# The fourth of each four products of h and its cosine on VectorE instead of GpSimd

## The chip, the cores and the metric

The kernel runs on one core of a Trainium2 chip, in float32 throughout. The metric is the device time of one execution in microseconds (us).

## The reference

Three stages follow one another. Attention keeps, in each row of scores, those that are at least the 32nd largest; its output is the input of a dense layer with a cosine gate; that layer's output goes through a mixture of eight experts, one per token.

```python
# attention: q, k, v are (4, 8, 576, 64)
scores = scale * np.matmul(q, k.transpose(0, 1, 3, 2))
kth = np.partition(scores, -top_k, axis=-1)[..., -top_k:-top_k + 1]   # top_k = 32
scores = np.where(scores >= kth, scores, -1000000000.0)
attn = np.exp(scores - np.max(scores, axis=-1, keepdims=True))
attn = attn / (np.sum(attn, axis=-1, keepdims=True) + 1e-09)
x = np.matmul(attn, v)                 # as (2304, 512)
# dense layer: w_in (512, 2048), w_out (2048, 512)
h = x @ w_in
x = (h * np.cos(h)) @ w_out
# experts: e = argmax(x @ w_gate); out = gate * sigmoid * (relu(x @ w1[e]) @ w2[e])
```

## The kernel before

Every engine has its own program, written out by hand, and they meet at semaphores. The work up to the experts is one loop of 75 steps (`LOOP`, 72 steps and a lag of three). Step `st` makes the scores of one tile of 128 queries for one pair of heads, four steps to a tile; the tiles that straddle two batches (steps 16 to 19 and 52 to 55) are "packed" and cost TensorE more. The stages of one step's data are spread over the following steps:

- in step `st` TensorE makes scores (L927, L933), ScalarE copies them from PSUM (L539), and VectorE finds the 32 largest of each row, for two heads: seven pairs of operations, op 0 to op 6, MAX8 (L728) at the even ones and MATCH_REPLACE8 (L730) at the odd ones;
- in step `st + 1` GpSimd turns the tops into constants (L407), ScalarE marks what lies below them (L525), GpSimd masks (L414, two instructions);
- in step `st + 2` ScalarE takes the exponentials (L533), GpSimd and VectorE make reciprocals of the sums (L419, L735), GpSimd multiplies by them (L424, two instructions);
- in step `st + 3` TensorE transposes the probabilities (L945, L952), ScalarE copies them (L547), TensorE multiplies them by v (L965 to L972), ScalarE copies the result into `x_T`.

Beside this runs the dense layer for the tokens of eight steps before, in blocks of two tiles, `m` = 0 to 7. `block_at(st)` gives the block and its place `i` = `st - (8m + 11)`, 0 to 9, so a block's i = 8 and 9 fall on the next block's i = 0 and 1. At i = 0 to 3 TensorE makes `h_T` (`hidden`, L983, 16 slices of 128 features by 256 tokens), in two parts of a step, with the transposes of the probabilities between them. At i = 2 and 4 VectorE reduces eight slices of h modulo 2 pi, `reduce_h`, in two operations: L743 behind op 1 and L746 behind op 2. ScalarE takes the absolute value (L591) at the end of that step and the sine (L596) in the next, each in two halves. At i = 3 and i = 5 GpSimd multiplies h by its cosine, in four products of two slices each (128 x 512 elements, `gate`, L434): pieces 0 to 3 of half g = 0 at i = 3, of half g = 1 at i = 5. They stand last in GpSimd's step, behind L424. At i = 4 to 7 TensorE multiplies the gated h by w_out (`outputs`, L994): features 0 to 7 of the first tile of tokens at i = 4 and of the second at i = 5, features 8 to 15 at i = 6 and 7, again in two parts of a step. Before every second feature it waits for the piece that holds it.

The last two tiles are done behind the loop in code of their own (L454, L602, L773, L1037, L1047), then come the routing on VectorE and the experts (L1108 to L1136), which the change does not touch.

Of the kernel before, what the change touches and what calls it, by code (L numbers as in the profile page):

```python
# [9 lines left out]
ALU = mybir.AluOpType  # L10
# [48 lines left out]
FULL = NT // BLOCK - 1  # L59
# [4 lines left out]
LAST = (NT - 2, NT - 1)  # L64
# [26 lines left out]
def block_at(s):  # L91

    return [(m, s - (8 * m + 8 + LAG)) for m in range(FULL) if 0 <= s - (8 * m + 8 + LAG) < 10]
# [45 lines left out]
def late_fill(t, quarter):  # L139
    return 4 * (t - LAST[0]) + quarter  # L140


def at_least(eng, sem, value):
    if value > 0:
        eng.wait_ge(sem, value)
# [9 lines left out]
def build(nc, q, k, v, w_in, w_out, w_gate, w_ogate, w1, w2, out):  # L155
# [4 lines left out]
    with ctx:  # L160
        def sb(name, shape, dt=F32, stack=ctx):
            return stack.enter_context(nc.sbuf_tensor(name, shape, dt))

        def sem(name):
            return ctx.enter_context(nc.semaphore(name))
# [59 lines left out]
        HS = sb("h_T", [P, NF, BT], stack=att)  # L225
        R = sb("reduced_h", [P, 2, NF // 2, BT], stack=att)
# [18 lines left out]

        names = ("ld_win ld_wout ld_wg const_ready small_filled small_emptied scores_done scores_copied "
                 "tops_done consts_done below_done masked_done exps_done den_done rden_done probs_ready probsT_done "
                 "probsT_copied dense_filled dense_emptied reduced_done cos_done gated_done late_filled late_emptied "
                 "route_chain sub_ready og_ready route_exp table_ready addr_ready "
                 "table_written rows_ready ids_cleared experts_loaded xgT_filled xgT_copied "  # L250
                 "eh_done relu_done ehT_done ehT_copied slot_done y_scaled tri_done oh_ready "
# [1 line left out]
        s = {n: sem(n) for n in names}  # L253
# [113 lines left out]
        def _(pool):  # L367
# [36 lines left out]
            def consts(u):  # L404
                pool.wait_ge(s["tops_done"], tops_at(u, 1, 6))
                at_least(pool, s["exps_done"], 2 * (u - 2))
                nc.gpsimd.tensor_tensor(TC[:, u % 3, :, :], TOP[:, u % 3, :, 0:TOPK:TOPK - 1],  # L407
                                        factors[:].unsqueeze(1).to_broadcast([P, 2, 2]), ALU.mult).then_inc(s["consts_done"], 1)

            def mask(u, i):  # L410

                pool.wait_ge(s["below_done"], 2 * u + i + 1)
                ex = EX[:, u % 3, i * S:(i + 1) * S]
                nc.gpsimd.tensor_tensor(ex, SS[:, u % 3, i, :], ex, ALU.subtract).then_inc(s["masked_done"], 1)  # L414

            def denominators(u):
                pool.wait_ge(s["exps_done"], 2 * u + 2)
                at_least(pool, s["rden_done"], u - 1)
                nc.gpsimd.tensor_scalar_add(DEN2[:, u % 2, :], DEN[:, u % 3, :], 1e-9).then_inc(s["den_done"], 1)  # L419

            def normalise(u):
                pool.wait_ge(s["rden_done"], u + 1)
                for i in range(2):
                    nc.gpsimd.tensor_scalar(EX[:, u % 3, i * S:(i + 1) * S], EX[:, u % 3, i * S:(i + 1) * S], RD[:, u % 2, i:i + 1], 1.0,  # L424
                                            ALU.mult, ALU.mult).then_inc(s["probs_ready"], 1)

            def gate(st, piece):

                for m, i in block_at(st):
                    if i in (3, 5):  # L430
                        g = (i - 3) // 2
                        f = g * 8 + piece * 2
                        pool.wait_ge(s["cos_done"], m * 8 + 4 * g + 2 + piece // 2 + 1)
                        nc.gpsimd.tensor_tensor(HS[:, f:f + 2, :], HS[:, f:f + 2, :], R[:, g, piece * 2:piece * 2 + 2, :],  # L434
                                                ALU.mult).then_inc(s["gated_done"], 1)

            for st in range(LOOP):
                if 0 <= st - 1 < NS:
                    consts(st - 1)
                if 0 <= st - 2 < NS:  # L440
                    denominators(st - 2)
                if 0 <= st - 1 < NS:
                    mask(st - 1, 0)
                    mask(st - 1, 1)
                if 0 <= st - 2 < NS:
                    normalise(st - 2)
                for piece in range(4):
                    gate(st, piece)

            for t in LAST:  # L450
# [262 lines left out]
        def _(dve):  # L713
            V = nc.vector

            def top_op(u, i, op):

                rnd = op // 2
                top = TOP[:, u % 3, i, rnd * 8:rnd * 8 + 8]
                src = SS[:, u % 3, i, :] if op < 2 else WK[:, i, :]  # L720
                if op == 0:
                    if i == 0:
                        dve.wait_ge(s["scores_copied"], u + 1)
                    at_least(dve, s["consts_done"], u - 2)
                else:
                    dve.wait_ge(s["tops_done"], tops_at(u, i, op - 1))
                if op % 2 == 0:
                    V.max(top, src).then_inc(s["tops_done"], 1)  # L728
                else:
                    V.match_replace(WK[:, i, :], top, src, NEG).then_inc(s["tops_done"], 1)  # L730
# [6 lines left out]
            def reduce_h(m, g, part):  # L737
                hs = HS[:, g * 8:(g + 1) * 8, :].rearrange("p a n -> p (a n)")
                r1 = R[:, g, :, :].rearrange("p a n -> p (a n)")
                if part == 0:  # L740
                    dve.wait_ge(s["dense_emptied"], m * MOE_FILLS + 8 * (g + 1))
                    at_least(dve, s["gated_done"], (2 * (m - 1) + g + 1) * 4)
                    V.tensor_scalar(r1.bitcast(I32), hs, 1.0 / TWO_PI, None, ALU.mult).then_inc(s["reduced_done"], 1)  # L743
                else:
                    dve.wait_ge(s["reduced_done"], m * 4 + 2 * g + 1)
                    V.scalar_tensor_tensor(out=r1, in0=r1.bitcast(I32), scalar=-TWO_PI, in1=hs,  # L746
                                           op0=ALU.mult, op1=ALU.add).then_inc(s["reduced_done"], 1)

            for st in range(LOOP):
                for op in range(7):  # L750
                    for i in range(2):
                        if st < NS:
                            top_op(st, i, op)
                        if op == 2 and i == 1 and 0 <= st - 2 < NS:
                            reciprocals(st - 2)
                    for m, i in block_at(st):
                        if i in (2, 4) and op in (1, 2):
                            reduce_h(m, (i - 2) // 2, op - 1)
# [8 lines left out]
            def late_reduce(t, g):  # L767
                n = FULL * 4 + (t - LAST[0]) * 4 + g * 2
                dve.wait_ge(s["late_emptied"], late_fill(t, 2 * g + 1) + 1)
                dve.wait_ge(s["gated_done"], FULL * 8 if t == LAST[0] else FULL * 8 + 2 * (g + 1))  # L770
                hs = HS[:, g * 8:(g + 1) * 8, t % 2 * P:t % 2 * P + P]
                r = R16[:, g * 8:(g + 1) * 8, :]
                V.tensor_scalar(r.bitcast(I32), hs, 1.0 / TWO_PI, None, ALU.mult).then_inc(s["reduced_done"], 1)  # L773
                dve.wait_ge(s["reduced_done"], n + 1)
                V.scalar_tensor_tensor(out=r, in0=r.bitcast(I32), scalar=-TWO_PI, in1=hs,
                                       op0=ALU.mult, op1=ALU.add).then_inc(s["reduced_done"], 1)
# [112 lines left out]
        def _(pe):  # L889
# [96 lines left out]
            def outputs(m, t, f0):  # L986
                if f0 == 0:
                    pe.wait_ge(s["dense_emptied"], m * MOE_FILLS + NF - 1 + t)
                    if m == 0 and t == 0:
                        pe.wait_ge(s["ld_wout"], 16)  # L990
                for f in range(f0, f0 + 4):
                    if f % 2 == 0:
                        pe.wait_ge(s["gated_done"], 8 * m + f // 2 + 1)
                    last = MM(HO[:, t, :], HS[:, f, t * P:(t + 1) * P], wout[:, f, :], start=f == 0, stop=f == NF - 1)  # L994
                if f0 == NF - 4:
                    last.then_inc(s["dense_filled"], 1)
# [44 lines left out]
            def late_outputs(t, f0):  # L1041
                if f0 == 0:
                    pe.wait_ge(s["dense_emptied"], y_fill(t - 2))
                for f in range(f0, f0 + 8):
                    if f % 4 == 0:
                        pe.wait_ge(s["gated_done"], FULL * 8 + (t - LAST[0]) * 4 + f // 4 + 1)
                    last = MM(HO[:, t % 2, :], HS[:, f, t % 2 * P:t % 2 * P + P], wout[:, f, :], start=f == 0, stop=f == NF - 1)  # L1047
                if f0 == 8:
                    last.then_inc(s["dense_filled"], 1)
# [134 lines left out]
```

## Time and profile before

| | |
|---|---|
| median of three runs | 1360.67 us (1356.54 to 1361.6) |
| the profiled execution | 1360.97 us |
| its span, first to last instruction | 1358.9 us |
| mean granted TensorE clock | 0.955 of full speed |
| TensorE matmuls busy | 1245.0 us, 92% |
| VectorE busy | 851.5 us, 63% |
| ScalarE busy | 641.1 us, 47% |
| GpSimd busy | 554.2 us, 41% |

The profiled execution lies 0.3 us above the median. 2.07 us of it lie outside the span. The loop fills the time from 13 to 869 us; VectorE's share of the whole span is low because it has little to do in the experts, and says nothing of the loop, which has to be read step by step.

### The profile page before, as it was taken

Reading aid. Unit: us, or ns where it says so; the run is one execution under the profiler, and the core shown is the slowest. Engines: PE = TensorE matmul, PEld = TensorE weight load, DVE = VectorE, ACT = ScalarE, POOL = GpSimd, SP = SyncE. Lnnn points to the kernel's source line nnn. Section 1 sums busy time; section 2 is a strip of 40 time slices with the busy share of each in tenths; the row PEclk is TensorE's granted clock in tenths of the full one; section 3 lists DMA queues with packets and bytes.
Section 4 is the critical chain, followed back from the end, with each engine's and each line's share of the span. In section 5 each row is a group of like instructions: output and inputs, shape, how many; then the busy total and the mean of one; then the engine's idle time right before and its main releaser. Section 6 shows DMA issues by size and latency. Waiting matters only on the chain. (4 is left out here: it accounts for less than half of the span.)

```text
span 1358.9 us, 18020 instructions
## 1 busy us (share of the span) xinstructions
PE 1245.0 (92%) x5962; PEld 792.3 (58%) x5963; DVE 851.5 (63%) x1690; ACT 641.1 (47%) x1082; POOL 554.2 (41%) x624
## 2 busy tenths in 40 slices
PE   4568999999999999999999999897599999999996
PEld 2446756857658668477577576584244444444443
DVE  6999996998998998988879989042211111111110
ACT  3555765775776766856757757340011111111110
POOL 2544662564754654735636636324211211112110
PEclk9667999999999999999999999898699999999998
DMA  7301001101001100100100000012414443251000
GB/s 239 115 9 26 9 26 26 34 9 34 9 25 35 26 24 1 26 25 18 44 24 1 8 9 1 16 68 73 144 33 155 158 149 143 74 190 70 15 14 1
DMA packets 81836, 71.49 MB, mean 53 GB/s; under 512 B 62266, under 2 KB 62266, under 8 KB 81248
## 3 DMA queue, kind: packets, MB, share of 16 engines
q1 hardware_dynamic: 76192, 60.86, 14.0%
q0 software_dynamic: 5568, 9.65, 2.2%
q8 instruction: 43, 0.70, 0.2%
q14 instruction: 33, 0.27, 0.1%
HBM read 62.97 MB, written 11.45 MB: 55 GB/s over the span
## 5 line engine op out<-in xcount | busy, mean ns | idle before, releaser
L728 DVE MAX8 tops<-scores_left 128x8 f32<-128x576 f32 x432 | 307.8, 762 | 0.0
L994 PE MATMUL dense_banks<-weights,h_T 128*128 128x512 f32 x512 | 235.5, 603 | 16.3 <-POOL h_T L434 16.3
L414 POOL TENSOR_TENSOR probs<-scores,probs 128x576 f32<-128x576 f32 x144 | 212.1, 1495 | 69.8 <-ACT probs L525 69.7
L983 PE MATMUL dense_banks<-x_T,weights 128*128 128x256 f32 x1024 | 234.9, 382 | 0.0
L730 DVE MATCH_REPLACE8 scores_left<-tops,scores_left 128x576 f32<-128x576 f32 x288 | 213.7, 757 | 0.0
L983 PEld LDWEIGHTS dense_banks<-x_T,weights 128*128 128x128 f32 x1024 | 189.4, 190 | 36.2 <-issue 13.1
L1136 PE MATMUL dense_banks<-weights,expert_h_T 128*128 x400 | 183.8, 592 | 0.0
L1117 PE MATMUL score_banks<-weights,x_gathered_T 128*128 x400 | 182.7, 600 | 1.0 <-DVE x_gathered_T L871 1.0
L994 PEld LDWEIGHTS dense_banks<-weights,h_T 128*128 128x128 f32 x512 | 93.0, 192 | 121.9 <-issue 95.8
L728 DVE MAX8 tops<-scores 128x8 f32<-128x576 f32 x144 | 102.4, 757 | 79.8 <-ACT scores L539 79.7
L424 POOL TENSOR_SCALAR probs<-probs,reciprocals 128x576 f32<-128x576 f32 x144 | 133.5, 938 | 6.0 <-DVE reciprocals L735 5.9
L876 DVE COPY expert_h_T<-dense_banks 128x512 f32<-128x512 f32 x25 | 17.3, 692 | 186.0 <-PE dense_banks L1127 186.0
L1117 PEld LDWEIGHTS score_banks<-weights,x_gathered_T 128*128 128x128 f32 x400 | 75.0, 193 | 86.3 <-issue 86.3
L525 ACT ACTIVATE probs<-scores,top_consts 128x576 f32<-128x576 f32 x144 | 103.5, 767 | 27.3 <-POOL top_consts L407 27.3
L1136 PEld LDWEIGHTS dense_banks<-weights,expert_h_T 128*128 128x128 f32 x400 | 72.2, 190 | 72.2 <-issue 72.2
L486 POOL DMA_INDIRECT out<-expert_y,slot_rows x25 | 25.7, 1027 | 216.5 <-ACT expert_y L699 216.5
L693 ACT ACTIVATE expert_h<-score_banks 128x512 f32<-128x512 f32 x50 | 29.9, 597 | 172.1 <-PE score_banks L1117 168.8
L533 ACT ACTIVATE probs<-probs,top_consts 128x576 f32<-128x576 f32 x144 | 110.4, 769 | 0.2
L539 ACT COPY scores<-score_banks 128x1152 f32<-128x1152 f32 x72 | 80.5, 1118 | 57.0 <-PE score_banks L933 44.5
L730 DVE MATCH_REPLACE8 scores_left<-tops,scores 128x576 f32<-128x576 f32 x144 | 106.6, 755 | 0.0
L699 ACT ACTIVATE expert_y<-dense_banks,slot_rows 128x512 f32<-128x512 f32 x25 | 17.2, 687 | 179.2 <-PE dense_banks L1136 179.2
L407 POOL TENSOR_TENSOR top_consts<-tops,top_factors 128x4 f32<-128x4 f32 x72 | 14.3, 198 | 204.6 <-DVE tops L728 204.6
(160 smaller groups left out, 1592.0 us busy)
## 6 DMA issues: line engine op xcount, KB each, us to landing
weights<-in_moe_w SPq DMA_DIRECT2D x16, 2048.0 KB, 10.9
y_rows<-y_rows_sb SPq DMA_DIRECT2D x18, 256.0 KB, 2.0
k_rows<-in_k SPq DMA_DIRECT2D x32, 128.0 KB, 2.6
q_rows<-in_q SPq DMA_DIRECT2D x16, 256.0 KB, 3.4
v_rows<-in_v SPq DMA_DIRECT2D x32, 128.0 KB, 2.3
weights<-in_moe_w_in SPq DMA_DIRECT2D x1, 4096.0 KB, 13.0
weights<-in_moe_w_out SPq DMA_DIRECT2D x1, 4096.0 KB, 23.2
k_rows<-in_k SPq DMA_DIRECT2D x16, 32.0 KB, 2.5
```

The lines of the kernel that those rows point to most:

```text
L414: nc.gpsimd.tensor_tensor(ex, SS[:, u % 3, i, :], ex, ALU.subtract).then_inc(s["masked_done"], 1)
L424: nc.gpsimd.tensor_scalar(EX[:, u % 3, i * S:(i + 1) * S], EX[:, u % 3, i * S:(i + 1) * S], RD[:, u % 2, i:i + 1], 1.0, ALU.mult, ALU.mult ...
L525: nc.scalar.activation(EX[:, a, i * S:(i + 1) * S], SS[:, u % 3, i, :], ACT.Relu, bias=TC[:, a, i, 1:2], scale=-BIG).then_inc(s["below_don ...
L533: nc.scalar.activation(ex, ex, ACT.Exp, bias=TC[:, a, i, 0:1], scale=SCALE, accum_out=DEN[:, a, i:i + 1]).then_inc(s["exps_done"], 1)
L539: copy(SS[:, st % 3, :, :].rearrange("p i n -> p (i n)").rearrange("p (a n) -> p a n", a=4), SPB[:, :, 0:HALF]).then_inc(s["scores_copied" ...
L693: nc.scalar.activation(HH[:, half * 512:(half + 1) * 512], SPB[:, half, :], ACT.Relu).then_inc(s["relu_done"], 1)
L728: V.max(top, src).then_inc(s["tops_done"], 1)
L730: V.match_replace(WK[:, i, :], top, src, NEG).then_inc(s["tops_done"], 1)
L983: last = MM(HO[:, f % 2, 0:BT], win[:, kd, f * P:(f + 1) * P], XT[:, m % 2, kd, :], start=kd == 0, stop=kd == KD - 1)
L994: last = MM(HO[:, t, :], HS[:, f, t * P:(t + 1) * P], wout[:, f, :], start=f == 0, stop=f == NF - 1)
L1117: last = MM(SPB[:, half, :], XGT[:, kd, :], WALL[:, bass.ds(expert % 2 * HALF_W + (kd * FE + half * 512), 512)], start=kd == 0, stop=kd == ...
L1136: last = MM(HO[:, 0, :], HT[:, f, :], WALL[:, bass.ds(expert % 2 * HALF_W + (KD * FE + f * DM), DM)], start=f == 0, stop=f == FEB - 1)
```

## The change

The products of piece 3 leave GpSimd, which keeps pieces 0 to 2, and go to VectorE as `gate_rest`, at the same places i = 3 and i = 5 of a block, between op 5 and op 6 of the step. VectorE waits there for the half's second sine (`cos_done`). Who waited for the fourth product waits for a new semaphore, `gated_rest`; the counts of the old one go from four to three a group. The two last tiles keep their own products on GpSimd.

```diff
-                for piece in range(4):
+                for piece in range(3):
                     gate(st, piece)
...
+            def gate_rest(m, g):
+
+                f = g * 8 + 6
+                dve.wait_ge(s["cos_done"], m * 8 + 4 * g + 4)
+                V.tensor_tensor(HS[:, f:f + 2, :], HS[:, f:f + 2, :], R[:, g, 6:8, :], ALU.mult).then_inc(s["gated_rest"], 1)
+
             for st in range(LOOP):
                 for op in range(7):
+                    if op == 6:
+                        for m, i in block_at(st):
+                            if i in (3, 5):
+                                gate_rest(m, (i - 3) // 2)
                     for i in range(2):
                         if st < NS:
                             top_op(st, i, op)
...
                 for f in range(f0, f0 + 4):
                     if f % 2 == 0:
-                        pe.wait_ge(s["gated_done"], 8 * m + f // 2 + 1)
+                        if f % 8 == 6:
+                            pe.wait_ge(s["gated_rest"], 2 * m + f // 8 + 1)
+                        else:
+                            pe.wait_ge(s["gated_done"], 6 * m + f // 8 * 3 + f % 8 // 2 + 1)
```

`reduce_h` and `late_reduce` wait for both semaphores before they write over the cosines, and the waits of the last two tiles count from `FULL * 6` instead of `FULL * 8`.

On VectorE, a block's steps i = 3 and the start of i = 4 stand so before (`tops` are the largest values, `scores_left` the scores with those taken out, `reduced_h` the argument of the cosine):

```order
L728 MAX tops<-scores 128x8 x2
L730 MATCH_REPLACE scores_left<-tops,scores 128x576 x2
L728 MAX tops<-scores_left 128x8 x2
L735 RECIPROCAL reciprocals<-denominators 128x2
L730 MATCH_REPLACE scores_left<-tops,scores_left 128x576 x2
L728 MAX tops<-scores_left 128x8 x2
L730 MATCH_REPLACE scores_left<-tops,scores_left 128x576 x2
L728 MAX tops<-scores_left 128x8 x2
L728 MAX tops<-scores 128x8 x2
L730 MATCH_REPLACE scores_left<-tops,scores 128x576 x2
L743 TENSOR_SCALAR reduced_h<-h_T 128x2048
```

and so with the change:

```order
L728 MAX tops<-scores 128x8 x2
L730 MATCH_REPLACE scores_left<-tops,scores 128x576 x2
L728 MAX tops<-scores_left 128x8 x2
L735 RECIPROCAL reciprocals<-denominators 128x2
L730 MATCH_REPLACE scores_left<-tops,scores_left 128x576 x2
L728 MAX tops<-scores_left 128x8 x2
L730 MATCH_REPLACE scores_left<-tops,scores_left 128x576 x2
L754 TENSOR_TENSOR h_T<-h_T,reduced_h 128x512
L728 MAX tops<-scores_left 128x8 x2
L728 MAX tops<-scores 128x8 x2
L730 MATCH_REPLACE scores_left<-tops,scores 128x576 x2
L744 TENSOR_SCALAR reduced_h<-h_T 128x2048
```

One product stands in front of the last pair of MAX8 of the step; nothing else has moved. On GpSimd, step i = 3 and the start of i = 4 of a block, before:

```order
L414 TENSOR_TENSOR probs<-scores,probs 128x576 x2
L424 TENSOR_SCALAR probs<-probs,reciprocals 128x576 x2
L434 TENSOR_TENSOR h_T<-h_T,reduced_h 128x512 x4
L407 TENSOR_TENSOR top_consts<-tops,top_factors 128x4
L419 TENSOR_SCALAR denominators<-sums 128x2
```

and with the change:

```order
L414 TENSOR_TENSOR probs<-scores,probs 128x576 x2
L424 TENSOR_SCALAR probs<-probs,reciprocals 128x576 x2
L434 TENSOR_TENSOR h_T<-h_T,reduced_h 128x512 x3
L407 TENSOR_TENSOR top_consts<-tops,top_factors 128x4
L419 TENSOR_SCALAR denominators<-sums 128x2
```

The group has three products instead of four, at the same place.

## Rows read from the trace of the kernel before

**Rows 1.** The page: busy time of the engines

```profile
PE 1245.0 (92%) x5962; PEld 792.3 (58%) x5963; DVE 851.5 (63%) x1690; ACT 641.1 (47%) x1082; POOL 554.2 (41%) x624
```

**Rows 2.** Waits of TensorE: whole program; then 434 to 526 us (total, times, longest)

```profile
PE dense_banks L994 <- POOL h_T L434: 16.3, 13, 2.3
...
PE dense_banks L994 <- POOL h_T L434: 2.5, 2, 1.5
PE small_banks L969 <- ACT probs_T L547: 0.6, 1, 0.6
```

**Rows 3.** Timeline of TensorE, blocks 1 and 3: start, duration, instructions, idle time before

```profile
291.99 3.70 PE L994 MATMUL dense_banks<-weights,h_T 128*128 128x512 f32 x8 [0.55 <-POOL h_T L434]
...
455.09 3.67 PE L994 MATMUL dense_banks<-weights,h_T 128*128 128x512 f32 x8 [1.01 <-POOL h_T L434]
...
474.60 0.49 PE L969 MATMUL small_banks<-probs_T,v_left 128*128 128x128 f32 x2 [0.64 <-ACT probs_T L547]
...
478.80 3.70 PE L994 MATMUL dense_banks<-weights,h_T 128*128 128x512 f32 x8 [1.51 <-POOL h_T L434]
```

**Rows 4.** Timeline of VectorE, block 3, i = 3 to i = 5

```profile
447.90 1.41 DVE L728 MAX8 tops<-scores 128x8 f32<-128x576 f32 x2
...
456.25 1.43 DVE L728 MAX8 tops<-scores_left 128x8 f32<-128x576 f32 x2
457.58 1.43 DVE L728 MAX8 tops<-scores 128x8 f32<-128x576 f32 x2
...
460.34 2.30 DVE L743 TENSOR_SCALAR reduced_h<-h_T 128x2048 int32<-128x2048 f32 x1
...
471.70 1.41 DVE L728 MAX8 tops<-scores 128x8 f32<-128x576 f32 x2
```

**Rows 5.** Timeline of GpSimd, block 3; the last row from 456.0 to 456.5 us alone

```profile
453.68 4.95 POOL L434 TENSOR_TENSOR h_T<-h_T,reduced_h 128x512 f32<-128x512 f32 x4
458.59 0.20 POOL L407 TENSOR_TENSOR top_consts<-tops,top_factors 128x4 f32<-128x4 f32 x1
...
471.87 0.20 POOL L407 TENSOR_TENSOR top_consts<-tops,top_factors 128x4 f32<-128x4 f32 x1 [4.31 <-DVE tops L728]
...
477.48 4.96 POOL L434 TENSOR_TENSOR h_T<-h_T,reduced_h 128x512 f32<-128x512 f32 x4
...
454.90 2.49 POOL L434 TENSOR_TENSOR h_T<-h_T,reduced_h 128x512 f32<-128x512 f32 x2
```

**Rows 6.** Durations by line, ns, minimum/median/maximum: L746, L743, L775, L434

```profile
L746 DVE SCALAR_TENSOR_TENSOR reduced_h<-reduced_h,h_T x16: 2265/2940/3481, 149.1 to 843.1; 128x2048 f32<-128x2048 int32 x16
...
L743 DVE TENSOR_SCALAR reduced_h<-h_T x16: 1217/1220/2298, 146.6 to 839.9; 128x2048 int32<-128x2048 f32 x16
...
L775 DVE SCALAR_TENSOR_TENSOR reduced_h<-reduced_h,h_T x4: 1224/1225/1226, 888.1 to 912.3; 128x1024 f32<-128x1024 int32 x4
...
L434 POOL TENSOR_TENSOR h_T<-h_T,reduced_h x64: 1257/1269/1282, 163.8 to 860.0; 128x512 f32<-128x512 f32 x64
```

**Rows 7.** Timelines of VectorE and GpSimd, block 3, i = 2, the reduction's second operation

```profile
438.95 3.48 DVE L746 SCALAR_TENSOR_TENSOR reduced_h<-reduced_h,h_T 128x2048 f32<-128x2048 int32 x1
...
437.25 3.02 POOL L414 TENSOR_TENSOR probs<-scores,probs 128x576 f32<-128x576 f32 x2 [1.82 <-ACT probs L525]
```

**Rows 8.** VectorE: waits, 434 to 526 us; starts of i = 8, block 3, and i = 4, block 5

```profile
DVE tops L728 <- ACT scores L539: 7.3, 4, 2.3
...
502.07 1.42 DVE L728 MAX8 tops<-scores 128x8 f32<-128x576 f32 x2 [1.18 <-ACT scores L539]
...
649.39 1.42 DVE L728 MAX8 tops<-scores 128x8 f32<-128x576 f32 x2 [5.97 <-ACT scores L539]
```

**Rows 9.** Timeline of TensorE, block 7; then 852 to 863 us by engine, PEclk the clock

```profile
853.75 0.49 PE L969 MATMUL small_banks<-probs_T,v_left 128*128 128x128 f32 x2 [1.69 <-ACT probs_T L547]
...
857.61 5.90 PE L994 MATMUL dense_banks<-weights,h_T 128*128 128x512 f32 x8 [2.34 <-POOL h_T L434]
...
852.00:863.00 11.00, 6.97 (x27) 3.48 (x27) 0.17 (x1) 8.23 (x12) 10.50 (x11) 0.69 0.00 0
```

More of the change, by code:

```diff
@@ L247, in build @@
                  "tops_done consts_done below_done masked_done exps_done den_done rden_done probs_ready probsT_done "
-                 "probsT_copied dense_filled dense_emptied reduced_done cos_done gated_done late_filled late_emptied "
+                 "probsT_copied dense_filled dense_emptied reduced_done cos_done gated_done gated_rest late_filled late_emptied "
                  "route_chain sub_ready og_ready route_exp table_ready addr_ready "
@@ L741, in reduce_h @@
                     dve.wait_ge(s["dense_emptied"], m * MOE_FILLS + 8 * (g + 1))
-                    at_least(dve, s["gated_done"], (2 * (m - 1) + g + 1) * 4)
+                    at_least(dve, s["gated_done"], (2 * (m - 1) + g + 1) * 3)
+                    at_least(dve, s["gated_rest"], 2 * (m - 1) + g + 1)
                     V.tensor_scalar(r1.bitcast(I32), hs, 1.0 / TWO_PI, None, ALU.mult).then_inc(s["reduced_done"], 1)
@@ L769, in late_reduce @@
                 dve.wait_ge(s["late_emptied"], late_fill(t, 2 * g + 1) + 1)
-                dve.wait_ge(s["gated_done"], FULL * 8 if t == LAST[0] else FULL * 8 + 2 * (g + 1))
+                dve.wait_ge(s["gated_done"], FULL * 6 if t == LAST[0] else FULL * 6 + 2 * (g + 1))
+                dve.wait_ge(s["gated_rest"], FULL * 2)
                 hs = HS[:, g * 8:(g + 1) * 8, t % 2 * P:t % 2 * P + P]
@@ L1045, in late_outputs @@
                     if f % 4 == 0:
-                        pe.wait_ge(s["gated_done"], FULL * 8 + (t - LAST[0]) * 4 + f // 4 + 1)
+                        pe.wait_ge(s["gated_done"], FULL * 6 + (t - LAST[0]) * 4 + f // 4 + 1)
                     last = MM(HO[:, t % 2, :], HS[:, f, t % 2 * P:t % 2 * P + P], wout[:, f, :], start=f == 0, stop=f == NF - 1)
```

## The prediction

> **What bounds the kernel now.** The page's first part has TensorE busy for 92% of the span and VectorE for 63% [rows 1]. That is a mean over stages, so I went on to the waits. In the eight steps from 434 to 526 us (block 3 from i = 2 to the next block's i = 2) TensorE waits three times: twice for GpSimd's products, 2.5 us in all, and once for ScalarE's copy of the probabilities, 0.6 us [rows 2]. Over the program it waits 13 times for the products, 16.3 us. A period takes 91.9 us. So TensorE works nearly throughout; the question is what ends those three waits.
>
> The timeline of TensorE puts them at the start of i = 4 (1.01 us, over at 455.09), in i = 5 (0.64, over at 474.60) and at the start of i = 6 (1.51, over at 478.80) [rows 3]. The timeline of GpSimd has its four products from 453.68 and again from 477.48 [rows 5]. One product is 1.27 us [rows 6], so the **first** of the four ends at 454.95 and at 478.75, 0.14 and 0.05 us before TensorE goes on. Neither wait is for the fourth.
>
> What ends the later waits is VectorE. The constants of i = 5, at 471.87, waited 4.31 us for the tops [rows 5]; the products follow 5.6 us behind them, through the marks, two masks and two normalisations. VectorE itself works without a gap from 447.90 to 471.70, where step i = 5 begins [rows 4]. The copy that TensorE waits for in i = 5 stands on ScalarE behind the marks of the same constants. So a period is made of two stretches: from the start of i = 2 to 478.80 VectorE sets the time, with the constants and products as its tail; from 478.80 to the scores of the next i = 2 TensorE does. Whatever is put on VectorE at i = 3 lies in the first stretch and is paid in full; what is put there at i = 5 lies beside the second.
>
> **The change part by part.** *Fourth product off GpSimd, 16 times, 1.27 us each.* Worth nothing: no wait of TensorE ends with it, and behind it GpSimd's next constants would have to wait for VectorE. At i = 3 they come at 458.59, at the end of the four products, and VectorE's tops are there at 457.68; the constants of the next step wait 4.31 us again.
>
> *The product on VectorE, by itself.* No such operation is in the loop. The nearest is the two-input reduction, 1.225 us for 1024 elements and 2.265 us for 2048 where nothing disturbs it [rows 6]: 1.04 us for each 1024, which makes 0.70 us for 512. In a row, instructions overlap: a pair of MAX8 of 1.43 us is followed after 1.33 [rows 4]. So 0.61 us.
>
> *The product on VectorE, beside GpSimd.* The reduction that starts at 438.95 takes 3.48 us in place of 2.27, so 1.22 more; GpSimd's masks, two-input operations too, ran from 437.25 to 440.27 [rows 7]. VectorE's operation was held until the running mask ended, 1.32 us later, less 0.10. At i = 3 the new product takes the place of the MAX8 at 456.25 [rows 4]. GpSimd's second and third product fill 454.90 to 457.39, the third from 456.13 [rows 5]: it starts 0.12 us ahead of VectorE and has 1.14 us to go. With the 0.10 off, VectorE is held for 1.04 us, and the product costs it 1.65. The bounds: 0.61, were VectorE first (then the third product is held, which nobody waits for), and 0.61 + 1.27 = 1.88 behind a whole product. I take 1.65, since both engines follow from the same tops of VectorE and their offset is fixed: at i = 5 VectorE is there at 471.70 + 8.35 = 480.05, and GpSimd's third product starts at 477.48 + 2.45 = 479.93, again 0.12 ahead [rows 4, 5].
>
> The Trainium skill (SBUF — State Buffer, "Who interferes with whom") states that a VectorE instruction with two SBUF inputs and a GpSimd one that reads SBUF exclude each other for the whole instruction. By that rule the wait is the full 1.14 us, and the sum would be 0.6 us higher; the row says 0.10 less, and I go by the row.
>
> *The next reduction.* At i = 4, L743 takes 2.30 us in place of 1.22 [rows 4, 6] for the same reason, a mask in its way. VectorE now comes to it 1.65 us later, the constants 0.8 us later (459.4 for 458.59), so that it meets the second mask near its start and not the first. Between 0 and a whole mask of 1.4 us; I take 1.2, which is 0.1 more than now. If the product cost only 0.61 us, L743 would come later against the first mask, be held 0.5 us in place of 1.08, and win all of it back. So the first stretch grows by 1.75 us, with 0 and 2.2 as its ends.
>
> *At i = 5.* The second product costs VectorE another 1.65 us. VectorE waits 1.18 us at i = 8 and 7.3 us in four steps of the period [rows 8]; this is its cover. The 0.5 us left over goes into the wait of the step behind. If the cover were gone, a period would take 1.65 us more.
>
> *Waits added.* VectorE waits for the second sine, with the last pair of MAX8, the next step's operations and then all constants queued behind it. GpSimd's third product needs the same sine, and starts at 456.13 with no idle time before it, so it is met when VectorE comes at 456.25: nothing. TensorE wants piece 3 in the second part of i = 4, behind the 3.67 us of matmuls that start at 455.09 [rows 3], and has it at 457.9: nothing.
>
> *The sum.* The 13 waits for products are two in each of the blocks 0, 2, 3, 4, 6 and 7 and one in block 1; block 7's are longer, the others like block 3's. Six blocks by 1.75 us are 10.5. In block 1 TensorE waits once, 0.55 us [rows 3]; I put the product alone, 0.6, between 0 and 1.75. Block 5 is the packed one: VectorE waits 5.97 us for scores right behind i = 3 [rows 8], so 0. In block 7's i = 5 no top-k is left; VectorE takes its product as soon as the sine is there, between GpSimd's first and second, and puts the second back by 0.6 us, for which TensorE waits there. Together 11.7 us, on the profiled execution's 1360.97: **1372.7 us**. That execution lies 0.3 us above the median of the runs shown, which I leave as it is.
>
> **The rivals.** *The product slips between GpSimd's, or L743 gives it back.* For it: 0.12 us decides who is first. Against: the offset is the same in every such block, and in rows 7 a lead of less than a tenth was enough. It gives 0 to 0.6 us a block, 1361 to 1365 us. Chance 0.18.
>
> *TensorE's clock falls.* In block 7 TensorE waits 1.69 us, then 2.34, and the next eight matmuls take 5.90 us in place of 3.70 (a part of that is a wait for the second product); the granted clock of that stretch is 0.69 [rows 9], so 0.62 of its time went at 1.2 GHz and the rest at 2.4. With the change the wait in i = 5 of blocks 2, 3, 4 and 6 goes from 0.64 to 2.4 us, with 1.51 behind it: as long together as block 7's. At up to 2.2 us in each of the four, 8.8 more: 1381.5 us. Against: much of a slow stretch would lie under the wait that follows. Chance 0.13.
>
> *GpSimd is the bound and is relieved: the other side.* The Trainium skill (GPSIMD Engine Reference, "Engine selection") gives elementwise work on two inputs to VectorE, with GpSimd about twice as slow; the trace agrees, 1.27 us against my 0.61. As a mechanism here: if the waits for products ended with the group and not with its first, each would shorten by up to 1.27 us. Of the 13 waits, 16.3 us, some 13.9 would go: 1347 us. It decides as soon as GpSimd comes late to its first product for a reason of its own. Against it are the 4.31 us that GpSimd waits for VectorE at the start of i = 5 [rows 5]. Chance 0.04.
>
> **How the numbers follow.** The forecast has 0.65, the rivals 0.18, 0.13 and 0.04. About 0.5%, 6.8 us, is what a measurement of this kernel can tell from no change. The forecast and the clock's rival are above it: slower 0.77. The slipping product is within it: same 0.19. Faster 0.04. The range goes from 1362, which takes in the upper part of the first rival and blocks at their lower end, to 1381.5, where six blocks at 2.2 us (1375) and some slow stretches lie. The likeliest case's own range is 1369 to 1377.
>
> **What the profile would show.** The product on VectorE at some 1.75 us in most of its 16 places, not 0.7; a period of 93.6 us where it is 91.9; TensorE's wait for the copied probabilities in i = 5 near 2.4 us in blocks 2, 3, 4 and 6, and those at i = 4 and i = 6 unchanged, still ended by the first product; block 5 as long as before; VectorE's wait at i = 8 gone. I would be wrong if the product took 0.7 us, if L743 lost its long cases, if the waits for L434 shrank, or if the granted clock fell in the middle blocks.

## The result, and the profile after

The changed kernel takes 1373.11 us (median of four runs, 1371.92 to 1375.01) against 1361.09 us for the kernel before beside it: a ratio of 1.0097, 95% interval 1.0071 to 1.0123. By the medians it is 12.0 us slower (their quotient is 1.0088); a ratio of 1.0097 would be 13 us; 1372.7 us was forecast. The executions of the kernel before lie up to 5.1 us apart, those of the changed one 3.1.

| | before | after |
|---|---|---|
| the profiled execution, us | 1360.97 | 1375.01 |
| its span, us | 1358.9 | 1373.4 |
| mean granted TensorE clock | 0.955 | 0.942 |
| VectorE busy, us | 851.5 | 875.5 |
| GpSimd busy, us | 554.2 | 531.3 |
| period, block 3's i = 2 to block 4's, us | 91.92 | 93.60 |

The period is the distance between the first MAX8 of two steps i = 2 on VectorE's timeline. Of the kernel before:

```profile
433.64 0.76 DVE L728 MAX8 tops<-scores 128x8 f32<-128x576 f32 x1 [2.25 <-ACT scores L539]
...
525.56 0.76 DVE L728 MAX8 tops<-scores 128x8 f32<-128x576 f32 x1 [1.70 <-ACT scores L539]
```

and of the changed kernel:

```profile
437.56 1.42 DVE L728 MAX8 tops<-scores 128x8 f32<-128x576 f32 x2 [2.25 <-ACT scores L539]
...
531.16 1.42 DVE L728 MAX8 tops<-scores 128x8 f32<-128x576 f32 x2 [1.70 <-ACT scores L539]
```

VectorE's timeline of the changed kernel, block 3, from i = 3 to the start of i = 5 (beside [rows 4]):

```profile
451.83 1.40 DVE L728 MAX8 tops<-scores 128x8 f32<-128x576 f32 x2
...
460.20 1.67 DVE L754 TENSOR_TENSOR h_T<-h_T,reduced_h 128x512 f32<-128x512 f32 x1
461.80 1.41 DVE L728 MAX8 tops<-scores_left 128x8 f32<-128x576 f32 x2
463.13 1.39 DVE L728 MAX8 tops<-scores 128x8 f32<-128x576 f32 x2
...
465.90 2.34 DVE L744 TENSOR_SCALAR reduced_h<-h_T 128x2048 int32<-128x2048 f32 x1
...
469.56 2.26 DVE L747 SCALAR_TENSOR_TENSOR reduced_h<-reduced_h,h_T 128x2048 f32<-128x2048 int32 x1
...
477.30 1.40 DVE L728 MAX8 tops<-scores 128x8 f32<-128x576 f32 x2
```

The new row is the product, L754: it takes 1.67 us, and the next instruction starts 1.60 us after it did. From i = 3 to i = 5 it is 25.47 us (477.30 less 451.83) where it was 23.80. GpSimd's timeline there (beside [rows 5]); the last row is from a look at 460.0 to 460.5 us alone:

```profile
457.60 3.73 POOL L434 TENSOR_TENSOR h_T<-h_T,reduced_h 128x512 f32<-128x512 f32 x3
463.29 0.20 POOL L407 TENSOR_TENSOR top_consts<-tops,top_factors 128x4 f32<-128x4 f32 x1 [1.96 <-DVE tops L728]
...
469.74 3.42 POOL L424 TENSOR_SCALAR probs<-probs,reciprocals 128x576 f32<-128x576 f32 x2 [2.58 <-DVE reciprocals L735]
477.46 0.20 POOL L407 TENSOR_TENSOR top_consts<-tops,top_factors 128x4 f32<-128x4 f32 x1 [4.31 <-DVE tops L728]
...
483.07 3.73 POOL L434 TENSOR_TENSOR h_T<-h_T,reduced_h 128x512 f32<-128x512 f32 x3
...
458.82 2.50 POOL L434 TENSOR_TENSOR h_T<-h_T,reduced_h 128x512 f32<-128x512 f32 x2
```

The group has three products, 3.73 us. The third runs from 460.06 to 461.32 (the last row's two products start at 458.82). VectorE's product comes at 460.20, while the third is running, so VectorE's is held, as forecast. Behind the group GpSimd now waits 1.96 us for VectorE's tops: what it was relieved of has become idle time. Durations by line, the product and the reduction's two operations (nanoseconds, minimum/median/maximum; beside [rows 6]):

```profile
L754 DVE TENSOR_TENSOR h_T<-h_T,reduced_h x16: 678/1673/1683, 167.1 to 871.6; 128x512 f32<-128x512 f32 x16
...
L744 DVE TENSOR_SCALAR reduced_h<-h_T x16: 1211/1218/2353, 147.3 to 853.9; 128x2048 int32<-128x2048 f32 x16
...
L747 DVE SCALAR_TENSOR_TENSOR reduced_h<-reduced_h,h_T x16: 2262/3464/3481, 149.8 to 857.5; 128x2048 f32<-128x2048 int32 x16
```

TensorE's waits in block 3 (timeline, beside [rows 3]), and ScalarE's two instructions ahead of the second of them:

```profile
459.01 3.67 PE L1009 MATMUL dense_banks<-weights,h_T 128*128 128x512 f32 x8 [1.01 <-POOL h_T L434]
...
474.92 1.09 PE L957 MATMUL score_banks<-ident,probs 128*128 128x128 f32 x8 [1.77 <-ACT scores L539]
...
480.19 0.49 PE L981 MATMUL small_banks<-probs_T,v_left 128*128 128x128 f32 x2 [0.64 <-ACT probs_T L547]
...
484.39 1.98 PE L1009 MATMUL dense_banks<-weights,h_T 128*128 128x512 f32 x4 [1.52 <-POOL h_T L434]
```

```profile
471.85 2.00 ACT L591 ACTIVATE reduced_h<-reduced_h 128x1024 f32<-128x1024 f32 x2 [3.19 <-DVE reduced_h L747]
473.76 1.10 ACT L539 COPY scores<-score_banks 128x1152 f32<-128x1152 f32 x1
```

There are four waits where there were three. Those of 1.01, 0.64 and 1.5 us are as before. The new one is 1.77 us in i = 5, in front of the transposes of the probabilities: it ends with ScalarE's copy of the scores at 474.86, which stands behind the absolute values, and those wait 3.19 us for VectorE's L747.

The blocks of the profiled executions, each from its i = 2 to the next one's, by the same differences on the timelines (us), with two of the experiments told of below:

```
block                 0       1      2      3      4       5      6
before           103.82   91.12  94.89  91.92  93.75  102.02  91.91
after            103.82   92.65  96.59  93.60  95.44  105.33  93.59
half g = 0 alone 103.81   92.66  96.59  93.59  95.43  102.02  93.60
half g = 1 alone 102.13   91.12  94.89  91.91  93.75  103.51  91.89
```

Blocks 2, 3, 4 and 6 are 1.68 to 1.70 us longer. The i = 2 of block 0 starts 0.7 us later, ahead of the first moved product, and over all the traces here it lies anywhere from 141.3 to 144.5 us; what follows the i = 2 of block 7 is 2.2 us longer. With the blocks that makes the 14.5 us between the spans. The profiled execution of the changed kernel lies 1.9 us above the median.

In blocks 0 and 5 the granted clock of TensorE plays a part. Here it is in the changed kernel for two stretches of block 5 (us, busy time of PE, PEld, DVE, ACT, POOL, then PEclk, the granted clock as a share of 2.4 GHz):

```profile
600.00:634.00 34.00, 34.00 (x221) 28.34 (x221) 28.61 (x56) 20.52 (x41) 13.47 (x17) 1.00 0.04 9
634.00:660.00 26.00, 22.77 (x132) 15.22 (x129) 17.66 (x35) 16.58 (x30) 11.67 (x12) 0.87 0.10 23
```

At 0.87 over 26 us, TensorE worked for 0.26 of them at 1.2 GHz, 6.8 us, and lost half of that: the 3.3 us by which the block is longer. The scores of a packed step show it: 16 matmuls in 3.82 us, where the same 16 take 2.16 us at 2.4 GHz (the second row is of half g = 1 alone, block 0).

```profile
637.56 3.82 PE L939 MATMUL score_banks<-k_T,q_T 64*64 64x288 f32 x16 [0.64 <-ACT k_T L575]
```

```profile
201.57 2.16 PE L941 MATMUL score_banks<-k_T,q_T 64*64 64x288 f32 x16 [0.64 <-ACT k_T L577]
```

What TensorE did ahead of the fall was short waits (0.56 and 0.64 us) around transposes of keys. They are not enough to explain it: the kernel before has the same two waits in front of the same scores at 630.27 us, and there the scores take 2.16 us. Over the eleven profiles of this study block 5 is 102.02 us in four, without a slow stretch, 103.5 to 103.7 in six, with one each, and 105.33 here with two. Block 0 is 103.82 us in the kernel before, with one slow stretch, and 102.13 without one in the run of half g = 1 alone, which leaves i = 3 as it was. The changed kernel has 103.82 without one. So the change costs block 0 about 1.69 us too, and the slow stretch happened to stay away.

### The profile page after: what moved, and what is told of

Its sections match the earlier page's. It is cut to its first block and busy times, and to the rows that moved or that the text cites. A ratio compares the mean times of both kernels' runs of the same rounds, so it can differ in the third digit from the quotient of the medians.

```text
span 1373.4 us, 18020 instructions
## 1 busy us (share of the span) xinstructions
PE 1252.0 (91%) x5962; PEld 796.7 (58%) x5963; DVE 875.5 (64%) x1706; ACT 641.8 (47%) x1082; POOL 531.3 (39%) x608
## 5 line engine op out<-in xcount | busy, mean ns | idle before, releaser
L728 DVE MAX8 tops<-scores_left 128x8 f32<-128x576 f32 x432 | 303.9, 743 | 0.0
L414 POOL TENSOR_TENSOR probs<-scores,probs 128x576 f32<-128x576 f32 x144 | 204.9, 1445 | 71.9 <-ACT probs L525 71.8
```

## The experiments

**Behind op 6.** VectorE comes to its product only when GpSimd's third one has ended.

```diff
 # the change's kernel
-                    if op == 6:
-                        for m, i in block_at(st):
-                            if i in (3, 5):
-                                gate_rest(m, (i - 3) // 2)
...
                         if i in (2, 4) and op in (1, 2):
                             reduce_h(m, (i - 2) // 2, op - 1)
+                        if op == 6 and i in (3, 5):
+                            gate_rest(m, (i - 3) // 2)
```

> The change with VectorE's product behind op 6 of the step, not in front of it. Theory (VectorE's time at i = 3 is paid, and most of it is the time in which the product is held by GpSimd's third): GpSimd's third product ends 9.5 us after the start of VectorE's step, and VectorE gets to its own at 9.7, so it takes 0.7 us and not 1.67. It shifts the next step's L743 by 0.6 us only, which is then held 0.5 us in place of 1.08 by the mask in its way: a period (i = 2 to i = 2, blocks 3 to 4) of 91.9 to 92.0 us in place of 93.6, total 1361 to 1363 us. Rival (TensorE waits for the fourth product, which VectorE delivers late): here it comes later still, so not under 1373 us.

Measured: 1359.39 us, ratio to the kernel before 1.0014 (1.0004 to 1.0023), period 91.92 us. The kernel before took 1358.09 us beside this run and the next three, 3 us less than beside the change, so the totals that I expected of them lie some 3 us high; ratios and periods are what compares. From its trace, the product and L744 (the reduction's first operation) by line, and the product and L744 of block 3 on VectorE's timeline:

```profile
L754 DVE TENSOR_TENSOR h_T<-h_T,reduced_h x16: 662/668/1159, 165.3 to 857.8; 128x512 f32<-128x512 f32 x16
...
L744 DVE TENSOR_SCALAR reduced_h<-h_T x16: 1205/1217/1670, 144.1 to 841.1; 128x2048 int32<-128x2048 f32 x16
```

```profile
456.67 0.67 DVE L754 TENSOR_TENSOR h_T<-h_T,reduced_h 128x512 f32<-128x512 f32 x1
...
460.04 1.66 DVE L744 TENSOR_SCALAR reduced_h<-h_T 128x2048 int32<-128x2048 f32 x1
```

The product is 0.67 us, and L744 is held 0.44 us in place of 1.08. The same work, on the same engine, 1.3 us later in the step, costs 0.14% and not 0.97%. TensorE does not wait for it: its three waits in block 3 are those of the kernel before.

**One half alone.**

```diff
 # the change's kernel; in the other run g == 1, i == 5
+                        if piece == 3 and g == 0:
+                            continue
...
-                            if i in (3, 5):
-                                gate_rest(m, (i - 3) // 2)
+                            if i == 3:
+                                gate_rest(m, 0)
```

GpSimd keeps the loop over four pieces, and the counts of the semaphores follow (not shown); the other run has `gate_rest(m, 1)`.

> The change for half g = 0 (i = 3) alone; at i = 5 GpSimd keeps its four products. Theory (what VectorE gets at i = 3 is paid, at i = 5 it lies beside TensorE's stretch): period 93.6 us, total 1371 to 1374 us. Rival (each product on VectorE costs alike): half of the change's 12 us, 1367 us.

Measured: 1369.27 us, ratio 1.0088 (1.0071 to 1.0104), period 93.59 us. The total lies 2 us under the range that I gave, where the kernel before was 3 us faster too; the ratio is nine tenths of the change's.

> The change for half g = 1 (i = 5) alone; at i = 3 GpSimd keeps its four products. Theory: period 91.9 us, the product on VectorE still 1.67 us, VectorE's wait of 1.18 us at i = 8 gone, total 1361 to 1363 us. Rival (each product on VectorE costs alike): 1367 us.

Measured: 1357.56 us, ratio 0.9995 (0.9986 to 1.0005), period 91.91 us. By line, the product of half g = 1 alone, and the start of i = 8 in block 3, where VectorE's wait of 1.18 us [rows 8] stood:

```profile
L756 DVE TENSOR_TENSOR h_T<-h_T,reduced_h x8: 869/1672/1678, 190.7 to 857.4; 128x512 f32<-128x512 f32 x8
```

```profile
499.82 1.41 DVE L730 MAX8 tops<-scores_left 128x8 f32<-128x576 f32 x2
501.15 1.40 DVE L730 MAX8 tops<-scores 128x8 f32<-128x576 f32 x2
```

The product is as dear (1.67 us) and costs nothing that can be told from no change. The wait at i = 8 is gone, 501.15 following its forerunner directly. So the two halves don't share the cost: in these blocks all of it is at i = 3.

**Time alone, without the product.** On the kernel before (the small tile and the semaphore that it needs are not shown):

```diff
+            def empty_reads(st):
+                if st < NS:
+                    dve.wait_ge(s["tops_done"], tops_at(st, 1, 5))
+                V.max(JUNK[:, 0:8], WK[:, :, :].rearrange("p a n -> p (a n)")).then_inc(s["junk_done"], 1)
+                V.max(JUNK[:, 8:16], WK[:, 0, 0:288]).then_inc(s["junk_done"], 1)
+
             for st in range(LOOP):
                 for op in range(7):
+                    if op == 6 and any(i in (3, 5) for m, i in block_at(st)):
+                        empty_reads(st)
```

> The kernel before, all four products on GpSimd, with two MAX8 over 1152 and 288 elements whose results nobody uses put on VectorE where the change puts its product: 1.6 us of VectorE's time that nothing of GpSimd can hold, no new semaphore for TensorE. Theory (only VectorE's time at i = 3 counts, neither the relief of GpSimd nor the new wait of TensorE): period 93.5 to 93.7 us, total 1371 to 1375 us, as the change. Rivals: if the wait for gated_rest were the cost, 1361 us; if GpSimd's relief hid a part of the cost, over 1376 us.

Measured: 1372.38 us, ratio 1.0092 (1.0066 to 1.0118), period 93.74 us. The reads take 1.76 us out of VectorE's step (11.44 us from start to start, 9.68 before), a little more than meant. The change's cost is there with all four products on GpSimd and no new semaphore for TensorE to wait for. The trace of this run has something more, TensorE in block 3's i = 5 and 6:

```profile
478.70 1.09 PE L954 MATMUL score_banks<-ident,probs 128*128 128x128 f32 x8 [1.91 <-ACT scores L540]
...
479.74 5.29 PE L1003 MATMUL dense_banks<-weights,h_T 128*128 128x512 f32 x8
...
488.19 3.70 PE L1003 MATMUL dense_banks<-weights,h_T 128*128 128x512 f32 x8 [0.73 <-POOL h_T L435]
```

The eight matmuls at 479.74 took 5.29 us, where they take 3.60 otherwise: a slow stretch of the clock behind the wait of 1.91 us. Yet this period of 93.74 us is no longer than that of block 6 of the same run, 93.76 us without a slow stretch: the wait for the copied probabilities (0.64 us) is missing and the one for the product is 0.73 in place of 1.51. This slow stretch lay ahead of waits that VectorE ends, and cost nothing.

**A short read in the same place.** One MAX8 over 512 elements in `empty_reads`, the rest as above.

> The kernel before with one MAX8 over 512 elements whose result nobody uses where the change puts its product: 0.6 us of VectorE's time that nothing can hold. Theory (L743 at i = 4 comes 0.6 us later against the mask that holds it, so it is held 0.5 us in place of 1.08): the 0.6 us at i = 3 are given back, period 91.9 to 92.0 us, total as before within 2 us. Rival (every bit of VectorE's time at i = 3 is paid): period 92.5 us, total 4 us over the kernel before.

Measured: 1361.34 us, ratio 1.0017 (1.0005 to 1.0029), period 91.91 us. VectorE's timeline, block 3:

```profile
455.09 0.69 DVE L753 MAX8 junk<-scores_left 128x8 f32<-128x512 f32 x1
...
459.79 1.55 DVE L744 TENSOR_SCALAR reduced_h<-h_T 128x2048 int32<-128x2048 f32 x1
```

The read takes 0.69 us, L743 (L744 here) takes 1.55 us where it took 2.30, and the period stands. That is the give-back that the forecast named for the lower end. It is not there in block 1, which is 92.79 us where it was 91.12. There, at i = 4, the reduction's second operation takes 3.47 us in place of 2.40:

```profile
274.62 3.47 DVE L747 SCALAR_TENSOR_TENSOR reduced_h<-reduced_h,h_T 128x2048 f32<-128x2048 int32 x1
```

Block 1 is 1.55 us longer in the run behind op 6 as well, which is most of that run's 0.14%.

**Twice the work.** GpSimd keeps two products a group, VectorE takes the other two as one operation; the counts of the semaphores follow (not shown).

```diff
 # the change's kernel
-                for piece in range(3):
+                for piece in range(2):
...
-                f = g * 8 + 6
+                f = g * 8 + 4
...
-                V.tensor_tensor(HS[:, f:f + 2, :], HS[:, f:f + 2, :], R[:, g, 6:8, :], ALU.mult).then_inc(s["gated_rest"], 1)
+                V.tensor_tensor(HS[:, f:f + 4, :], HS[:, f:f + 4, :], R[:, g, 4:8, :], ALU.mult).then_inc(s["gated_rest"], 1)
```

> The change with the third and fourth product of each group on VectorE, as one operation of 128 x 1024 at the change's place in front of op 6; GpSimd keeps two. Theory (it is GpSimd's third product, started 0.12 us ahead, that makes the change dear, not the work moved): GpSimd is through with its second product at 8.2 us of VectorE's step and VectorE comes at 8.4, so the doubled operation takes 1.2 us and not 1.67, and L743, 1.1 us later in the next step, comes at the end of the mask that holds it now and gives up to 1.0 us back: period 91.9 to 92.3 us, total 1359 to 1364 us. Rival (what VectorE gets there is paid by its amount, once and for all): twice the product's own time, period 93.0 us or more, 8 us over the kernel before.

Measured: 1355.63 us against 1353.09 us of the kernel before on that chip, ratio 1.0020 (1.0010 to 1.0030), period 91.99 us. The total was given for another chip's level; ratio and period are what compares. The product and L744 by line:

```profile
L754 DVE TENSOR_TENSOR h_T<-h_T,reduced_h x16: 1202/1208/1681, 166.4 to 861.2; 128x1024 f32<-128x1024 f32 x16
...
L744 DVE TENSOR_SCALAR reduced_h<-h_T x16: 1206/1217/2362, 146.5 to 843.5; 128x2048 int32<-128x2048 f32 x16
```

1.21 us for 1024 elements, where the change pays 1.67 for 512. Twice the work on VectorE costs a fifth of what the change costs. Most of it is given back: L744 at i = 4 of block 3 takes 1.21 us, where it took 2.30.

The traces of these runs, put side by side, show what makes the price. Block 3, VectorE's steps i = 3 and i = 4 from start to start, with the reduction's first operation (L743 or L744) at i = 4 (us):

```
                    step i = 3   first operation   step i = 4   period
before                    9.68              2.30        14.12    91.92
product behind op 6      10.29              1.66        13.50    91.92
short read               10.41              1.55        13.38    91.91
two products             10.84              1.21        13.04    91.99
the change               11.31              2.34        14.17    93.60
long reads               11.44              2.35        14.17    93.74
```

Up to 1.16 us more at i = 3 the reduction's hold shrinks by about as much, and the period stands to 0.07 us. With 1.63 us more it starts while the second mask runs (465.90, the mask from 465.75 to 467.16) and is held as before, and all of the time is paid. Between 1.16 and 1.63 us no run lies. So the hold by GpSimd's third product, 1.0 us, costs 1.68: it is paid itself, and it takes the product's own 0.6 us out of what would have been given back.

**The reduction's second operation at i = 2 later.** This spends the same insight on what was already there: L746 was held by a mask in every block [rows 7].

```diff
 # the kernel before
-                        if i in (2, 4) and op in (1, 2):
-                            reduce_h(m, (i - 2) // 2, op - 1)
+                        if i in (2, 4) and op == 1:
+                            reduce_h(m, (i - 2) // 2, 0)
+                        if op == (4 if i == 2 else 2) and i in (2, 4):
+                            reduce_h(m, (i - 2) // 2, 1)
```

> The kernel before with the second operation of the reduction at i = 2 (L746 there) behind op 4 in place of op 2. Theory (VectorE from i = 2 on sets the first stretch, and this operation is held 1.22 us by a mask): GpSimd's normalisations are over when VectorE gets to it, so it takes 2.27 us and not 3.48: VectorE's step i = 2 is 13.0 us in place of 14.3, period (blocks 3 to 4) 90.7 us in place of 91.9, total 7 to 10 us under the kernel before. Rival (the absolute value and the copy of the scores behind it on ScalarE, on which TensorE's transposes wait, come 1.6 us later and take the gain back): no difference to the kernel before.

Measured: 1351.29 us against 1360.5 us, ratio 0.9940 (0.9920 to 0.9960), period 90.59 us. It beats both kernels. The reduction's two operations by line, and TensorE's waits from 429 to 520 us (one period):

```profile
L746 DVE SCALAR_TENSOR_TENSOR reduced_h<-reduced_h,h_T x16: 2271/2336/2402, 150.9 to 835.0; 128x2048 f32<-128x2048 int32 x16
...
L743 DVE TENSOR_SCALAR reduced_h<-h_T x16: 1214/1217/1220, 145.6 to 832.5; 128x2048 int32<-128x2048 f32 x16
```

```profile
PE dense_banks L996 <- POOL h_T L434: 0.9, 1, 0.9
PE dense_banks L985 <- ACT h_T L563: 0.6, 1, 0.6
PE score_banks L947 <- ACT scores L539: 0.5, 1, 0.5
```

L746 is at most 2.40 us, where half of its 16 cases took 3.48. The 1.33 us of the period do not come from that place alone. In block 3 VectorE's step i = 2 is 13.43 us in place of 14.26 (I had expected 13.0), step i = 3 is 10.11 in place of 9.68, and step i = 4 is 13.19 in place of 14.12, because L743 is no longer held there: 1.22 us at all 16 places. I had not foreseen this second gain. The rival was partly there: TensorE now waits 0.5 us for the copy of the scores behind the later absolute values. At 0.5 us it does not take the gain back.

**Two that missed.** The last edit with the fourth products on VectorE behind op 6:

> The last edit together with all sixteen fourth products on VectorE behind op 6. Theory: as the last one within 2 us, since the product behind op 6 costs VectorE 0.6 us at i = 3 and L743 gives as much back. Rival (with VectorE's stretch shorter, GpSimd's group is the next bound, and being one product shorter is worth something): 2 to 8 us under the last one.

Measured: 1366.79 us, ratio 1.0055 (1.0034 to 1.0076), period 92.60 us. Neither the theory nor the rival: it is 15.5 us over the last edit alone. Timelines of VectorE and of GpSimd in block 3, i = 3:

```profile
460.20 1.53 DVE L754 TENSOR_TENSOR h_T<-h_T,reduced_h 128x512 f32<-128x512 f32 x1
```

```profile
457.45 3.73 POOL L434 TENSOR_TENSOR h_T<-h_T,reduced_h 128x512 f32<-128x512 f32 x3
```

The sine comes later with the reduction, GpSimd's group starts 7.0 us into VectorE's step and not 5.8, and its third product runs until 461.18: the place behind op 6 is no longer free, the product takes 1.53 us, and L743 is held again, 2.30 us.

And L743 behind op 0 at both places, L746 at i = 2 behind op 4:

> The kernel before with the first operation of the reduction (L743) behind op 0 in place of op 1, at both places, and the second at i = 2 behind op 4. Theory (the hold of L743 at i = 4, 1.08 us, is paid as well): L743 runs before the masks start and takes 1.22 us at all 16 places; period 89.7 to 90.2 us, total 14 to 18 us under the kernel before. Rival (TensorE becomes the bound once its three waits, 3.2 us a period, are partly gone, or GpSimd's products do): no more than the 7 to 10 us of the edit with the second operation alone.

Measured: 1360.83 us, ratio 1.0007 (0.9997 to 1.0018), period 91.67 us: no gain, 9.5 us worse than the later reduction alone. VectorE's and GpSimd's timelines in i = 4:

```profile
455.89 1.59 DVE L743 TENSOR_SCALAR reduced_h<-h_T 128x2048 int32<-128x2048 f32 x1
...
460.25 3.10 DVE L746 SCALAR_TENSOR_TENSOR reduced_h<-reduced_h,h_T 128x2048 f32<-128x2048 int32 x1
```

```profile
453.89 2.50 POOL L434 TENSOR_TENSOR h_T<-h_T,reduced_h 128x512 f32<-128x512 f32 x2
...
458.43 2.77 POOL L414 TENSOR_TENSOR probs<-scores,probs 128x576 f32<-128x576 f32 x2 [0.59 <-ACT probs L525]
```

L743, early, falls on GpSimd's fourth product and is held 0.37 us; L746, with it, on the second mask and is held 0.84. TensorE was not the bound: its wait of 1.51 us at i = 6 is there. The theory had a wrong premise: the hold of 1.08 us that this edit was to win was already gone with the later reduction alone, where L743 takes 1.22 us everywhere. So there was nothing left to win at L743, and the move brought two new holds.

## Why the prediction was right

*What bounds the kernel.* Right. Two stretches, VectorE's from i = 2 to the product that TensorE waits for at i = 6, TensorE's from there: the half at i = 3 alone makes the period 93.59, the half at i = 5 alone leaves it at 91.91.

*The product by itself*, 0.61 us from start to start, 0.70 in duration: 0.67 us in the run behind op 6.

*The product beside GpSimd*, 1.65: it is 1.60 from start to start. Which engine was first, the point on which the forecast hung, came out as the offset of 0.12 us said (0.14 in the trace), in each of the six blocks that I had counted.

*The next reduction*, 0.1 more than now: 2.34 us where it was 2.30, so 0.04. The two together lengthen the period by 1.68 us where I had 1.75.

*At i = 5*, cover enough: right. *Fourth product off GpSimd*, nothing: right, it waits 1.96 us for the tops instead.

*The sum*, 11.7, is 12.2 without the clock's part: 1.69 for block 0, 1.53 for block 1, 6.75 for blocks 2, 3, 4 and 6, 2.2 from block 7 on (I had 2.35). Of block 7's part 2.0 us are there in the run of half g = 0 alone, where I had 1.75, and 0.3 in that of half g = 1 alone, where I had 0.6. Block 0's second wait for a product was 0.60 us in the kernel before and not 1.51 as in block 3, which I had overlooked; the block lengthened like the others all the same. One term was mis-sized by more than that: block 1, which I put at 0.6 us. VectorE's timeline there, the changed kernel and then the kernel before:

```profile
270.95 0.68 DVE L754 TENSOR_TENSOR h_T<-h_T,reduced_h 128x512 f32<-128x512 f32 x1
...
278.17 3.46 DVE L747 SCALAR_TENSOR_TENSOR reduced_h<-reduced_h,h_T 128x2048 f32<-128x2048 int32 x1
```

```profile
277.01 2.40 DVE L746 SCALAR_TENSOR_TENSOR reduced_h<-reduced_h,h_T 128x2048 f32<-128x2048 int32 x1
```

The product itself is 0.68 us, since here VectorE came first, and GpSimd's third product was held in its place; the longest of the 48 in the change:

```profile
L434 POOL TENSOR_TENSOR h_T<-h_T,reduced_h x48: 1260/1270/1728, 164.5 to 873.6; 128x512 f32<-128x512 f32 x48
```

The Trainium skill (SBUF — State Buffer, "Who interferes with whom") has the order of issue decide which of the two engines is held. The trace agrees: 0.09 us behind VectorE's, GpSimd's product took 1.73 us and not 1.27. So step i = 3 of block 1 is only 0.48 us longer. But coming that much later, the reduction's second operation at i = 4 found the second mask running and was held by all of it, 3.46 us in place of 2.40. That is the other 1.06 us. It takes no product to bring it about: the short idle read, which leaves GpSimd's four products alone, has the same 3.47 us and makes block 1 1.67 us longer. I had put the product's own time there and not asked what the next reduction would meet. Block 5, which I put at 0, is as long as before in the run of the first half alone; its 3.3 us in the profiled execution are the clock's, and block 0's slow stretch, 1.7 us, went at the same time.

*The number.* That 1373.11 us lies within 0.4 us of 1372.7 is in part luck. Block by block the terms agree to 0.15 us but for block 1, 0.9 us too low; the executions of one kernel lie 3 to 5 us apart; and the profiled ones differ by 14 us. The chances of the forecast and of the clock's rival, both slower, add up to 0.78, where I wrote 0.77.

*What the profile would show.* The period of 93.6 us, 1.67 us for most products, and VectorE's wait at i = 8 gone: right. One step failed. I had the delay reach TensorE through the copy of the probabilities, with that wait going from 0.64 to 2.4 us. It reaches TensorE earlier in the same step through the reduction's second operation (L747 now), the absolute values and the copy of the scores, as a new wait of 1.77 us, and the 0.64 us stays. Before, that path was just met: the copy of the scores ended at 469.27, TensorE's matmuls ahead of it at 469.22, so no wait showed. The sum does not change, because either way TensorE waits for the same VectorE.

*The rivals.* The product did not slip in front of GpSimd's third one but in block 1, and there it did not make the block cheap. That GpSimd is relieved and the kernel gains did not happen. The clock's rival was put in blocks 2, 3, 4 and 6, and there the clock stayed at 1.00 in the changed kernel; where it did fall in such a place, with the idle reads, the waits behind it took it up. Where it cost something was block 5, at which I had not looked. Whether it falls there differs between runs with the same waits of TensorE, and what decides it was not tried, so how much of the 3.3 us the change has to answer for stays open.

## What to carry to other kernels

Here a product that started on VectorE in the middle of one of GpSimd's took its own time and what was left of GpSimd's, less 0.1 us. What it then cost hung on the next operation that was held: up to 1.16 us came back there, 1.63 us did not. So before work is moved from GpSimd to VectorE, put VectorE's new start beside GpSimd's operations of that moment, and then the start of the next operation that is held beside what it will meet. Here an offset of 0.12 us made 0.6 us into 1.6, a place 1.3 us later made it free in all blocks but one, and the gain to be had (9 us) was in operations that were already held in the kernel before. Look at what the first of a group releases before shortening the group's end, and after every such shift look again at the neighbours: two of three further moves by the same reasoning ran into the next one, and the third gained at a place that had not been reckoned with.

## What the runs showed that I had not expected

The work moved and the time paid can go opposite ways: 1024 elements on VectorE cost 0.07 us a period, 512 cost 1.68. A wait of zero can hide a path that is just met, as the copy of the scores was. And TensorE's clock, on the same work of TensorE, made block 5 102.0, 103.5 to 103.7 or 105.3 us long, in steps as large as the differences between executions of one kernel (1356.54 to 1361.6 us for the kernel before); whether those differences are this was not tried.
